# A fused attention and two-MLP kernel: the opening chunks in another order, and the gather of the second MLP ahead of its scatter

## The reference

```python
for t in range(S):                       # attention, each (b, h)
    cur = outer(u * k[t], v[t])
    y[t] = r[t] @ (state + cur)
    state = w[t][:, None] * state + outer(k[t], v[t])

h = x @ w_in                             # first MLP
x2 = maximum(0.01 * h, h) @ w_out

logits = normalize(x2) @ normalize(expert_emb).T / tau    # second MLP
expert_idx = argmax(logits)              # one expert a token, gate = its softmax
out[mask] = gate * (maximum(x2[mask] @ w1[e], 0.0) @ w2[e])
```

## Time and profile before

| What | Value |
|---|---|
| median of the runs | 853.58 us |
| the profiled execution, its own time | 855.45 us |
| its span | 853.7 us |
| PE busy | 824.6 us (97%) |
| DVE, ACT, POOL busy | 550.9, 439.1, 203.3 us |
| first feature matmul starts | 41.03 us |
| one tile of the second MLP on PE | 9.59 us |
| last matmul ends | about 845.7 us |

### The profile page before, as it was taken

How to read it: one execution, slowest core, us unless ns; L and a number is a source line. 1 busy time by engine, 2 the same in 40 slices (tenths; PEclk the granted TensorE clock), 3 DMA queues, 4 the chain that set the end, 5 groups by cost and what they waited for, 6 DMA issues and landing times.

```text
span 853.7 us, 17833 instructions
## 1 busy us (share of the span) xinstructions
PE 824.6 (97%) x5689; PEld 775.1 (91%) x5689; DVE 550.9 (65%) x1296; ACT 439.1 (51%) x919; POOL 203.3 (24%) x285
## 2 busy tenths in 40 slices
PE   5789999999999999999999999999999999999995
PEld 4689999999999999999999999999989998989885
DVE  5587688678878778778878865645361412455472
ACT  3565464464465456446447435554563533565472
POOL 5421001012112112112112001213342323334443
PEclk9899999999999999999999999999999999999999
DMA  8795221127232112122120000513531513386381
GB/s 164 156 228 152 52 66 39 35 73 87 45 79 39 39 34 66 38 42 66 39 51 29 2 15 29 168 38 86 200 124 37 182 46 112 116 272 205 117 274 50
DMA packets 141575, 78.80 MB, mean 92 GB/s; under 512 B 111566, under 2 KB 129525, under 8 KB 141362
## 3 DMA queue, kind: packets, MB, share of 16 engines
q1 hardware_dynamic: 135794, 65.73, 30.7%
q0 software_dynamic: 4544, 10.85, 3.8%
q10 hardware_dynamic: 1152, 1.18, 0.6%
HBM read 112.90 MB, written 11.63 MB: 146 GB/s over the span
## 4 chain that ended last, share of the span: by engine, by line
PE 90%; issue 1%; DMA 1%; DVE 1%; ACT 0%; POOLq 0%; POOL 0%; DVEq 0%; ACTq 0%; SPq 0%
PE bank L996 24%; PE bank L975 23%; PE bank L1048 13%; PE bank L1084 13%; PE bank L872 3%; PE bank L904 3%; PE bank L1065 3%; PE bank L932 3%; PE bank L927 2%; PE bank L912 1%; PE bank L1030 1%; PE bank L941 1%; DMA stage<-in_moe_w_dram 1%; PE bank L1021 0%; DMA xg<-x_moe,gi 0%
## 5 line engine op out<-in xcount | busy, mean ns | idle before, releaser
L975 PE MATMUL bank<-xhl,WRh 128*128 128x384 f32 x768 | 219.7, 340 | 1.3 <-DMA xhl<-xhl 1.3
L1317 ACT COPY gw<-bank 128x384 f32<-128x384 f32 x128 | 61.6, 481 | 162.8 <-PE bank L975 162.6
L975 PEld LDWEIGHTS bank<-xhl,WRh 128*128 128x128 f32 x768 | 142.3, 189 | 1.6 <-DMA xhl<-xhl 1.6
L996 PE MATMUL bank<-WRh,gh 128*128 128x384 f32 x384 | 136.6, 356 | 0.0
L975 PE MATMUL bank<-xhl,WRl 128*128 128x384 f32 x384 | 130.7, 340 | 0.0
L996 PE MATMUL bank<-WRh,gl 128*128 128x384 f32 x384 | 129.9, 338 | 0.0
L996 PE MATMUL bank<-WRl,gh 128*128 128x384 f32 x384 | 129.7, 338 | 0.0
L1596 DVE SCALAR_TENSOR_TENSOR gw<-gw 128x384 f32<-128x384 f32 x128 | 71.5, 559 | 62.5 <-ACT gw L1317 62.5
L1603 DVE TENSOR_TENSOR gl<-gw,gh 128x384 fp32r<-128x384 f32 x128 | 79.6, 622 | 46.2 <-ACT gh L1323 43.9
L1323 ACT CAST gh<-gw 128x384 fp32r<-128x384 f32 x128 | 65.4, 511 | 70.3 <-DVE gw L1596 58.4
L1771 DVE TENSOR_TENSOR hl<-bank,hh 128x512 fp32r<-128x512 f32 x56 | 36.1, 686 | 85.6 <-ACT hh L1358 85.2
(11 more groups left out here) (191 smaller groups left out, 1647.6 us busy)
## 6 DMA issues: line engine op xcount, KB each, us to landing
stage<-in_moe_w_dram SPq DMA_DIRECT2D x96, 768.0 KB
Wn<-in_w_dram SPq DMA_DIRECT2D x24, 192.0 KB, 2.6
Rn<-in_r_dram SPq DMA_DIRECT2D x24, 192.0 KB, 3.4
Kn<-in_k_dram SPq DMA_DIRECT2D x24, 192.0 KB, 3.6
Vn<-in_v_dram SPq DMA_DIRECT2D x24, 192.0 KB, 3.3
x_moe<-x2s SPq DMA_DIRECT2D x24, 192.0 KB, 2.6
wraw<-in_moe_w_out_dram SPq DMA_DIRECT2D x4, 768.0 KB, 7.8
eraw<-in_moe_w_dram SPq DMA_DIRECT2D x4, 768.0 KB, 7.9
```

Source lines behind the costliest of these rows:

```text
L975: mm = pe.matmul(bank[F_BANK[n % 2]][:, 0:GN], win(t_)[:, f // 4, k_, cols], xhl[G % 2][:, a, k_, :], start=(k_ == 0 and n_ == 0), stop=(k ...
L996: mm = pe.matmul(bank[O_BANK[i]][:, 0:DM], a[:, z, cols], wout(t_)[:, f, :], start=(f == 0 and n_ == 0), stop=(f == FT - 1 and n_ == 2))
L1317: act.copy(gw[:, n % 2, :], bank[F_BANK[n % 2]][:, 0:GN]).then_inc(s_g0, 1)
```

## The change

Three things are altered.

**1. The opening.** SyncE no longer waits for GpSimd's fill of the padding before its first load, and w has semaphores of its own (`s_natw`), so that `turn_w` waits for w alone and `turn_rk` for r and k. The r loads of chunks 0 to 2 and the load of u are issued by ScalarE. VectorE has another order: `bonus_sum(m)` ahead of `decay_rk(m)`, both masks ahead of `decay_w(2)`, and `decay_w` is cut in `decay_to` (forward scans) and `decay_from` (the rest), with `decay_to(3)` ahead of the first MLP. `FL` is written by a `tensor_reduce` over one element in place of a `tensor_copy`, for every chunk. ScalarE does `check_decays` ahead of `diagonal`, and `split_hi(0)` earlier.

**2. The holes of group 0.** The six DMAs go. ScalarE copies the last pair of heads to SBUF (`y_rows`, 128x128), and TensorE adds its rows into the holes with six matmuls a chunk (`move_rows`, 64x64 by 64x128, with a shifted identity in `moves`). `y_hi` and `y_lo` of those chunks write 384 columns in place of 512. The first feature waits for `s_yhi` and `s_ylo` in place of `s_fill`. TensorE's `warm(20)` goes and `warm(14)` becomes `warm(18)`. On GpSimd `products(3)` stands ahead of `state(2)`. Later groups keep the DMAs.

**3. The second MLP.** From tile 5 on GpSimd's `tile` does `fetch(j + 3)` first, then scatter, `drain` and the copies. `drain(n)` scatters the last result ahead of its wait for the gathers. SyncE loads the list ahead of the weights.

```diff
-            sp.wait_ge(s_const, 1)
-            load(0)
-            load(1)
-            sp.dma_start(ub[:], ...)
+            load(0, 2)
+            load(1, 2)
             load_v(0)
-            load(2)
+            load(2, 2)
...
             load_weights(1)
-            fill(0)
-            sp.wait_ge(s_fill, 16 * 2 * KT)
             sp.dma_start(taub[:], tau.rearrange("(a n) -> a n", a=1).to_broadcast([P, 1])).then_inc(s_tau, 16)
...
             def step(j, s_, half):
+                if not whole(j) or j + 3 < MT:
+                    load_ids(j + 3, 1 - s_)
                 if not whole(j) or j + 1 < MT:
                     weights(j + 1)
-                if not whole(j) or j + 3 < MT:
-                    load_ids(j + 3, 1 - s_)
...
             def tile(j, s_, half):
+                first_tiles = whole(j) and j < K1
+                if not first_tiles and (not whole(j) or j + 3 < MT):
+                    fetch(j + 3, 1 - s_, half + 1 + s_)
                 if not whole(j) or j > 0:
                     scatter_out(j - 1, 1 - s_, s_out[1 - s_])
                 if not whole(j) or j > K1:
...
             def drain(n):
+                scatter_out(n - 1, (n - 1) % 2, s_last)
                 for i in range(2):
                     pool.wait_ge(s_xg[i], 16 * ((min(n + 3, MT) + 1 - i) // 2))
-                scatter_out(n - 1, (n - 1) % 2, s_last)
...
+            def move_rows(m):
+                c_ = banks(m)[2]
+                pe.wait_ge(s_perm, 2)
+                pe.wait_ge(s_y3, m + 1)
+                for k_ in range(KT):
+                    for o in range(2):
+                        rows = slice(o * HEAD_PAD, (o + 1) * HEAD_PAD)
+                        mm = pe.matmul(bank[c_][rows, k_ * P:(k_ + 1) * P], moves[rows, k_, :], y3[rows, :],
+                                       start=False, stop=True, skip_group_check=True)
+                mm.then_inc(s_pm, 1)
...
+            def y_rows(m):
+                act.wait_ge(s_ym, m + 1)
+                if m > 0:
+                    act.wait_ge(s_pm, m)
+                act.copy(y3, pair(banks(m)[2])[:, KT, :]).then_inc(s_y3, 1)
...
-                dve.tensor_copy(FL[:, m % GT, :], Fi[:, z, :, P]).then_inc(s_fl, 1)
+                dve.tensor_reduce(FL[:, m % GT, :], Fi[:, z, :, P:P + 1], AX.X, ALU.max).then_inc(s_fl, 1)
```

More of the change, by code:

```diff
@@ L191, in build @@
         bonus = sb("bonus", [P, 2, H], c=att)
+        s_natw = [sem(f"s_natw{i}") for i in range(NSLOT)]
         s_nat = [sem(f"s_nat{i}") for i in range(NSLOT)]
@@ L216, in build @@
         s_bo = sem("s_bo")
+        s_y3 = sem("s_y3")
+        s_pm = sem("s_pm")
+        s_perm = sem("s_perm")
+        s_bias = sem("s_bias")
         att.close()
@@ L792, in tile @@
                 pool.tensor_copy(gcol[:, s_, :], idall[:, bass.ds(j, 1), 1]).then_inc(s_gate, 1)
[L793 to L796, removed]
+                if first_tiles:
+                    if j + 3 < K1:
+                        gather(j + 3)
+                    else:
+                        fetch(j + 3, 1 - s_, half + 1 + s_)
             def mlp(first, lo, hi):
@@ L1156, in _ @@
             turn_w(2)
-            warm(14, EARLY[2][1])
+            warm(18, EARLY[2][1])
             scores(1)
@@ L1160, in _ @@
             turn_rk(2)
+            move_rows(0)
             sums(1)
             scores(2)
+            turn_w(GT)
+            move_rows(1)
             sums(2)
-            turn_w(GT)
+            move_rows(2)
             turn_rk(GT)
-            warm(20, EARLY[0][1])
             mlp(0, 0, SECOND)
@@ L1233, in y_hi @@
                     act.wait_ge(s_h, FT * (g - 1))
-                act.copy(xhl[g % 2][:, 0, :, i * P:(i + 1) * P], pair(banks(m)[2])).then_inc(s_yhi, 1)
+                if g == 0:
+                    act.wait_ge(s_pm, m + 1)
+                nk = KT + 1 if g else KT
+                act.copy(xhl[g % 2][:, 0, 0:nk, i * P:(i + 1) * P], pair(banks(m)[2])[:, 0:nk, :]).then_inc(s_yhi, 1)
+            def y_rows(m):
[3 more added lines that the diff above has]
+                act.copy(y3, pair(banks(m)[2])[:, KT, :]).then_inc(s_y3, 1)
             def fill(g):
@@ L1458, in start_moe @@
                     tile(j, j % 2, j // 2)
-            act.wait_ge(s_const, 3)
-            act.activation(junka[:, 0:1], nbias[:, 0:1], ACT.Copy, scale=ones[:, 0:1]).then_inc(s_warm, 1)
-            act.wait_ge(s_warm, 1)
+            act.wait_ge(s_bias, 1)
+            act.activation(junka[:, 0:1], nbias[:, 0:1], ACT.Copy, scale=nbias[:, 1:2]).then_inc(s_warm, 1)
+            load_one(act, 0, 1)
+            act.dma_start(ub[:], u.rearrange("(a h) d -> a (h d)", a=1).to_broadcast([P, DM])).then_inc(s_small, 16)
+            load_one(act, 1, 1)
+            load_one(act, 2, 1)
+            act.wait_ge(s_warm, 1)
+            act.wait_ge(s_const, 3)
+            act.wait_ge(s_perm, 1)
+            for o in range(2):
+                rows = slice(o * HEAD_PAD, (o + 1) * HEAD_PAD)
+                ins = act.copy(moves[rows, :, D:HEAD_PAD],
+                               ident[rows, o * HEAD_PAD:o * HEAD_PAD + D].rearrange("p (k i) -> p k i", k=KT))
+            ins.then_inc(s_perm, 1)
+            check_decays(0)
             diagonal(0)
-            check_decays(0)
             back(0)
+            check_decays(1)
             diagonal(1)
+            split_hi(0)
+            y_rows(0)
+            back(1)
             y_hi(0)
-            back(1)
-            split_hi(0)
             diagonal(2)
+            y_rows(1)
             y_hi(1)
-            check_decays(1)
             back(2)
+            y_rows(2)
             y_hi(2)
-            fill(0)
             split_hi(1)
@@ L1884, in _ @@
             state_sum(1)
+            mask(2)
             y_lo(1)
-            mask(2)
-            y_lo(2)
+            decay_to(GT)
             state_sum(2)
             bonus_sum(GT)
+            y_lo(2)
             mlp(0, 0, SECOND)
```

62 lines of the change are left out of this document (40 added, 22 removed).

## The result

The changed kernel takes 840.9 us, the median of four runs (839.8 to 841.1), against 853.82 (852.83 to 854.3) for the kernel before in the same comparison: 12.9 us less, a ratio of 0.9848 [0.983 to 0.9865]. The forecast was 837.1 with a range of 833 to 843.5, so the time is in that range, but 0.9 outside the forecast's own narrower range of 834 to 840, and 3.6 us of the forecast gain of 16.5 did not come. The profiled execution of the changed kernel takes 839.8 us with a span of 838.0; the one of before took 855.45.

What follows compares the result with a forecast made beforehand. TensorE was taken as the bound except in the opening, until about 53 us, and at the end. Gains of 8.8 + 4.2 + 3.5 = 16.5 off the median 853.58 gave 837.1, range 833 to 843.5 (8 in 10).

Steps and rivals of the forecast that it cites:

- The start: Opening: earlier loads and w awaited alone bring the first transpose to 5.1 and first scan to 6.3, 2.2 us earlier.
- `Kt(2)` 2.2 us earlier: VectorE's opening: reordered bonus and masks and no `FL` stall end chunk 2's `Kt` at 24.2, 2.2 us before today's.
- First feature 8.8 us earlier: Opening: from `Kt(2)` to the first feature 8.0 us in place of 14.65, so it comes at 32.2 instead of 41.03.
- about 2.5 of lower clock: Opening, TensorE: share of the 14.65 us before the first feature put down to the lower clock, expected to go.
- The loads, at nothing: Opening: weights quarter 0 and chunk 3's w there at about 21, wanted at 26; margin 3 to 5 us, no cost.
- rival (b): Opening: loads or ScalarE's queue late by 5 beyond the margin, gain 11.5, time 842.1; chance 0.10.
- First steps: First to fourth feature: the wait for `Kt(3)` and the slow piece go, 12.6 us become 8.4, saving 4.2.
- The end: Last tile: the last scatter follows the last scaling by 0.94 us instead of a gather's landing, 3.5 us earlier.
- (a): Opening: TensorE's clock falls once or twice, 1.6 to 3.2 us each; with longer hops gain 12, time 841.6; chance 0.17.
- (c): End: last scatter not earlier because the queue is the wait, not the gather; gain 13, time 840.6; chance 0.06.
- (d): Second MLP: gather ahead of scatter holds up each tile, 23 us per us over, 863.6 at 1 us; chance 0.02.
- (e): Opening does not move because something unseen holds the first feature; only the end gains, time 850.1; chance 0.03.

Runs made afterwards that it cites:

- b3: Changed kernel with the first loads as before, all on SyncE after the padding, u behind six tensors, w's own semaphores kept: 845.33 us, ratio 0.9904.
- b2: Changed kernel with `FL` written by a `tensor_copy` again in place of the reduce: 844.08 us, ratio 0.9892.
- a2: Kernel before with only the second MLP part of the change: 850.84 us, ratio 0.9954.
- d1: Changed kernel with the first loads as before on SyncE, but u issued by ScalarE first of all: 840.64 us, ratio 0.9842.
- b4: Changed kernel with chunk 3's forward scans back in the first step of the MLP: 839.98 us, ratio 0.9844.
- c1: Changed kernel with `split_lo(3)` moved behind `state_sum(3)` on VectorE: 839.59 us, ratio 0.9828.
- a1: Changed kernel run again without any edit: 840.37 us, ratio 0.9832; the kernel before beside it took 853.91.
- b1: Changed kernel with group 0's holes filled by the six DMAs again, 512 columns and `warm(20)` back: 844.54 us, ratio 0.9896.
- a4: Changed kernel with the old tile order (scatter ahead of `fetch`, weights ahead of the list), new `drain` kept: 844.96 us, ratio 0.9896.
- a3: Changed kernel with the old order in `drain` (wait for the gathers, then last scatter), new tile order kept: 840.93 us, ratio 0.9839.

## Why the prediction was right or wrong

**The start, 2.2 us: right**, 2.24, but the reason was half right. The step gave both the earlier loads and w's own semaphore a part; b3 has the loads of before and loses 0.14 of it. The transpose waited for the triangle, at 5.06, as forecast (5.1).

**`Kt(2)` 2.2 us earlier: right**, 2.3 (23.39 + 0.68 = 24.07 against 26.38). The stall of `FL` is gone in every chunk. It was sized 0.64 + 2.3 us from two stalls of before; b2 shows that it is worth more in the new order, 3.7 us, since the stall there falls in a place where TensorE has nothing else and the clock falls with it. On the rule of the Trainium skill (SBUF — State Buffer, "Who interferes with whom") b2 agrees, with the copy ending within 0.03 us of GpSimd's product, and the reduce taking 0.13.

**First feature 8.8 us earlier: right in the profile**, 9.3, with 7.6 us from `Kt(2)` where 8.0 were forecast. (The working there is loose by 0.2 and 0.3: its terms up to y of chunk 2 add up to 29.2 where it has 29.35, and those from 30.0 on to 31.9 where it has 32.2.) But the term held "about 2.5 of lower clock", and this is the first step that failed: not its mechanism, its size. It was read from one execution in which the stretch at 0.50 lasted 6.4 us. a2, with the same opening, has 3.2 us of it and a first feature 1.7 earlier. I then took the whole gain, 16.5, off the median of 853.58, as if the 1.9 us between that median and the profiled execution had nothing to do with the opening. The slow stretch goes away whole, so the time after is the same whether it had been long or short, and an execution with the short one gains less. The profiled execution less the gain, 838.9, was the consistent forecast, and that profile gave 839.8.

**The loads, at nothing: nearly right for the changed kernel's profile, wrong as a rule.** The step had the weights there at about 21 and wanted at 26. Their high part is wanted much earlier: `split_hi(0)` is ready for it at 17.6 (19.15 less its wait of 1.59) and stands ahead of `y_rows(0)`, as rival (b) said. TensorE's wait for it is 0.63 in the changed kernel and up to 1.40 in the traces with the same opening, where it moves the first feature by up to 0.7. What the Trainium skill (DMA: Bandwidth & Descriptors, "Issuing engines are not separate DMA queues") says of a second queue no run here shows by itself, since b3 and d1 put back the queue and the time of issue together. But the place of u in the order was part of the change, and I cost it at nothing where, with the bonus sum moved ahead of `Kt(0)`, it carries 5 us. Two edits that I priced one by one hung on each other.

**First steps, 4.2 us: right up to the fourth feature and wrong behind it.** To the fourth feature the trace has 8.1 us after 12.6, which is 4.5 saved. Then 1.1 is given back. The step said that VectorE "stays just ahead" with 16.6 us of work in 18. It does not: `leak(0)` takes 1.96 us beside GpSimd's L722 (0.56 in b4, where it comes as L722 ends), and `split_lo(3)` stands ahead of the state that TensorE needs. c1 takes that wait away by moving one instruction. A sum of work against a window says nothing about the one result inside the window that is due early.

**The end, 3.5 us: right in the mechanism**, and the scatter is 0.92 after the scaling as forecast (0.94). The time behind the scatter grew by 0.6, so 3.0 came in the profile, and 3.1 in a2 by medians.

**The rivals.** (a) The clock never fell in the changed kernel's two traces. (b) The weights were late for ScalarE as it said, but by 0.3 to 1.4 us on TensorE and not by 5 beyond a margin. (c) The last scatter was earlier. (d) No wait for `os` came; the new tile order was a gain. (e) The opening moved.

**The account.** In the profiled pair: 13.8 in the opening, less 1.1 for VectorE, plus 3.5 for the scatter, less 0.6 behind it, makes 15.7 with rounding (forecast 16.5). The pair of a1 and a2, which share one comparison, has medians 10.5 apart, and their traces 10.6 at chunk 4's r transposes (59.52 and 48.91); the pair of profiles on which I built has 12.7 there. So about 2 of the missing us are a draw of which execution was profiled. Where that enters the medians can be written down, though it is the same numbers once more and no second proof: in a1's comparison the profiled execution of before is 1.5 above its median and the one of the changed kernel 0.6 below, and 15.7 less these is the 13.5 measured. In the first comparison they are 1.6 above and 1.1 below, which makes the 12.9. The median lies inside the stated range by its width: the range was drawn so wide for rivals that did not come in that form, and what did happen, the choice of the execution, was not among them. That much is luck. The openings of the other runs of the kernel before (851.9 to 857.8 over all comparisons) were not traced, so how often each length of the low clock occurs stays open.

## What to carry to other kernels

When a change removes a stretch at the lower clock, its length in one profiled execution is a draw and not a constant: take the forecast off that same execution, or look at a second trace first. Price together the edits that hang on each other: an instruction moved ahead on a busy engine needs its input earlier, and one load issued behind six others cost more (5.0 us) than any other edit here was worth. After a wait is removed, list which result on each helper engine is due first, not only how much work it has; and on GpSimd's side let one queue's gathers go before the scatter that must wait anyway.

## What the runs showed of the hardware

- The same instructions behind the same kind of gap (2.8 us) left TensorE's granted clock at 0.50 for 3.2 us in one execution and 6.4 in another. Gaps of 2.67 (b1), 3.10 (b2) and 3.81 us (b3) were followed by 3.4 us at 0.54, by four at 0.62 and by about seven near 0.50.
- A VectorE copy of 128x4 took 2.73 us beside a GpSimd product of 3.45, and a `SCALAR_TENSOR_TENSOR` of 128x384 1.96 in place of 0.56. A `TENSOR_REDUCE` of the same 128x4 took 0.13 in the same place.
- From the issue of the last scatter to the end of the span passed 3.0 to 4.5 us in kernels whose last gather was long done or had just landed, and 5.4 with a gather issued 1.4 us ahead of it (a4, one execution).
- Six DMAs inside SBUF that move a few rows took 4.1 us (before) and 4.35 us (b1) from the last write of the data to the first matmul on it.
- The same load of weights let ScalarE start at 18.84 to 19.93 us in five traces of kernels with one and the same opening (changed, a1, a3, a4, c1), which moved the first feature from 31.69 to 32.35.
